# Twelve expert layers after attention on one NeuronCore: the first projection as seven block products in place of eight, tokens in two groups of 768

## The reference

```python
def _moe_ref(x, domain_probs, w1, w2) -> np.ndarray:
    ...
    p = domain_probs / (domain_probs.sum(-1, keepdims=True) + 1e-09)
    for e in range(E):
        h = np.maximum(x @ w1[e], 0.0)
        out += p[:, e:e + 1] * (h @ w2[e])

def _moe2_ref(x, w_gate, w1, w2) -> np.ndarray:
    ...
    logits = x @ w_gate
    logits = logits - logits.max()
    P = np.exp(logits)
    for _ in range(8):
        P /= P.sum(1, keepdims=True) + 1e-09
        P /= P.sum(0, keepdims=True) + 1e-09
        P *= N / E
    for e in range(E):
        h = np.maximum(x @ w1[e], 0.0)
        ye = h @ w2[e]
        out += P[:, e:e + 1] * ye
```

## Time and profile before

| | us |
|---|---|
| median of 3 runs | 1688.06 (1685.53 to 1688.75) |
| span of the profiled execution | 1684.4 |
| PE busy in it | 1651.6 |
| DVE busy | 489.4 |
| ACT busy | 322.8 |
| POOL busy | 35.3 |

### The profile page before, as it was taken

The page is one execution under the profiler, slowest core; times in us unless marked ns, Lnnn a source line. Parts: engine busy times, 40 slices in busy tenths (PEclk is TensorE's granted clock), DMA queues, the critical chain, the costliest instruction groups (busy, mean ns, idle before and its releaser), DMA issues.

```text
span 1684.4 us, 19145 instructions
## 1 busy us (share of the span) xinstructions
PE 1651.6 (98%) x8037; PEld 1363.8 (81%) x8037; DVE 489.4 (29%) x811; ACT 322.8 (19%) x551; POOL 35.3 (2%) x39
## 2 busy tenths in 40 slices
PE   6799999999999999999999999999999999999999
PEld 5778888888888887888888888888888888888887
DVE  5541321231231242272132132123123123123212
ACT  4631221121121131121121121112112112112110
POOL 2310000000000000000000000000000000000000
PEclk9799999999999999999999999999999999999999
DMA  8950020020020011002002002002002001100001
GB/s 188 147 167 1 0 100 1 1 100 0 0 99 0 0 50 51 1 3 98 1 0 100 0 0 100 0 0 100 0 0 99 0 0 59 40 0 0 8 17 50
DMA packets 50964, 66.56 MB, mean 40 GB/s; under 512 B 27880, under 2 KB 27880, under 8 KB 50928
## 3 DMA queue, kind: packets, MB, share of 16 engines
q1 hardware_dynamic: 50928, 66.04, 13.5%
HBM read 62.89 MB, written 3.15 MB: 39 GB/s over the span
## 4 chain that ended last, share of the span: by engine, by line
PE 94%; SPq 3%; issue 1%; DVE 1%; ACT 0%; DMA 0%; POOL 0%; POOLq 0%
PE banks L356 31%; PE banks L355 31%; PE banks L357 31%; SPq L187 1%; SPq L186 1%; PE banks L435 0%; DMA v_bd<-in_mem_v 0%; SPq L193 0%; SPq L189 0%; PE banks L316 0%; DVE acc L755 0%; PE banks L406 0%; PE banks L408 0%; PE banks L395 0%; SPq L169 0%
## 5 line engine op out<-in xcount | busy, mean ns | idle before, releaser
L706 DVE SCALAR_TENSOR_TENSOR h_lo<-banks,h_hi 128x512 fp32r<-128x512 f32 x288 | 199.0, 691 | 1130.0 <-ACT h_hi L571 1130.0
L356 PE MATMUL banks<-w_hi,h_hi 128*128 128x512 f32 x1152 | 453.8, 394 | 0.0
L355 PE MATMUL banks<-w_lo,h_hi 128*128 128x512 f32 x1152 | 451.9, 392 | 1.4 <-DVE x_lo L714 1.4
L355 PE MATMUL banks<-x_lo,w_hi 128*128 128x512 f32 x1152 | 448.8, 390 | 0.2
L356 PE MATMUL banks<-x_hi,w_hi 128*128 128x512 f32 x1152 | 448.2, 389 | 0.0
L357 PE MATMUL banks<-x_hi,w_lo 128*128 128x512 f32 x1152 | 447.9, 389 | 0.0
L357 PE MATMUL banks<-w_hi,h_lo 128*128 128x512 f32 x1152 | 447.4, 388 | 0.0
L571 ACT ACTIVATE h_hi<-banks 128x512 fp32r<-128x512 f32 x288 | 171.9, 597 | 1300.7 <-PE banks L357 1300.7
L355 PEld LDWEIGHTS banks<-w_lo,h_hi 128*128 128x128 f32 x1152 | 216.3, 188 | 50.9 <-DVE x_lo L714 1.8
L357 PEld LDWEIGHTS banks<-w_hi,h_lo 128*128 128x128 f32 x1152 | 216.2, 188 | 48.3
L355 PEld LDWEIGHTS banks<-x_lo,w_hi 128*128 128x128 f32 x1152 | 216.2, 188 | 47.3 <-DVE x_lo L744 0.7
(11 more groups left out here) (82 smaller groups left out, 297.4 us busy)
## 6 DMA issues: line engine op xcount, KB each, us to landing
w_raw<-in_moe_w SPq DMA_DIRECT2D x24, 2048.0 KB, 8.1
v_bd<-in_v SPq DMA_DIRECT2D x16, 308.0 KB
w_raw<-in_q SPq DMA_DIRECT2D x8, 384.0 KB, 5.0
w_raw<-in_k SPq DMA_DIRECT2D x8, 384.0 KB
out_x<-acc SPq DMA_DIRECT2D x12, 256.0 KB, 2.1
v_bd<-in_mem_v SPq DMA_DIRECT2D x16, 48.0 KB
v_bd<-in_v SPq DMA_DIRECT2D x16, 10.0 KB
v_bd<-in_v SPq DMA_DIRECT2D x16, 12.0 KB
```

The costliest lines, as they stand in the source:

```text
L355: pe.matmul(out_, lhs_hi, rhs_lo, start=start, stop=False)
L356: pe.matmul(out_, lhs_hi, rhs_hi, start=False, stop=False)
L706: dve.scalar_tensor_tensor(out=h_lo[:, f % 4, :], in0=h_ps[f % 4], scalar=0.0, in1=h_hi[:, f % 4, :].bitcast(F32), op0=ALU.max, op1=ALU.su ...
```

## The change

The first projection is done in blocks of 2 by 2: halves of the contraction (256 each), two chunks of hidden columns (128 each), halves of a batch (384 tokens each). With Strassen's scheme (Winograd's variant of it) seven block products give what eight would give; each product takes a sum or difference of weight blocks (`s`) as the stationary operand and one of token blocks (`t`) as the moving one. A quad is such a pair of hidden chunks for one batch: 42 matmuls with a moving operand of 384 columns, where the old order takes 48 for the same work with 384 each, or 36 with 512. 96 quads make up the program: batch 0 through the first mixture (quads 0 to 15), batch 1 (16 to 31), batch 0 through the second (32 to 63), batch 1 (64 to 95). All of it is written out, without loops.

- The seven products of a quad go to four banks of PSUM (`CHAIN`, `OPENS`): some are added by TensorE in the bank itself, and four partial sums are copied out by ScalarE (`keep_part`) and added back in PSUM by VectorE (`add`, 128x384) before the ReLU.
- GpSimd makes the sums of the weight blocks (`sum_s`, four operations of 256 columns a quad) and those of the tokens (`sum_t`, `sum_t4`, four of 768 columns a pass). ScalarE and VectorE split all seven weight blocks of a quad at once (1792 columns).
- `w1_raw` now holds one quad: the next quad's blocks are loaded with two transfers of 256 KB in rows of 512 bytes, when VectorE has split the last.
- The second projection is done by halves of an expert (4 chunks), in 24 pieces (tile, chunk) that are put between the products of the next two quads (`PIECES`). The output is accumulated twice an expert, in place of once.
- The chunks of expert 0 no longer stand in the attention. The logits are taken with the transposed rows as the stationary operand and 8 moving columns, 48 full-precision products in all.
- The eight rounds of the gates stand three to a quad, in quads 35 to 37.

```diff
+STATIONARY = (1, 2, 4, 3, 5, 0, 6)
+PRODUCTS = 7
+CHAIN = (0, 1, 0, 3, 0, 2, 3)
+OPENS = (True, True, False, True, False, True, False)
+PIECES = (2, 2, 1, 2, 2, 2, 1)
...
+    PASSES = 2 * B
+    FIRST = [0, EA, 2 * EA, 2 * EA + EB, 2 * EA + 2 * EB]
+    JOBS = FIRST[PASSES]
...
+        LAST_A = [4 * FIRST[b + 1] for b in range(B)]
+        TURNS = {}
+        for t in range(ST):
+            TURNS[LAST_A[0] + 2, t] = ("turn", 0, t)
+        TURNS[LAST_A[0] + 2, 6] = ("logits", 0, 0)
+        for t, (dq, i) in enumerate(((1, 0), (1, 1), (1, 2), (1, 4), (2, 0), (2, 1))):
+            TURNS[LAST_A[1] + dq, i] = ("turn", 1, t)
+        TURNS[LAST_A[1] + 2, 3] = ("logits", 1, 0)
+        SINK0 = LAST_A[1] + 3
...
+            def load_w1(quad):
+                n, j = quad // QUADS, quad % QUADS
+                src = weights(n)[0].rearrange("(c p) f -> p c f", p=P)
+                if quad:
+                    sp.wait_ge(s_lo_ready, quad)
+                for odd in (1, 0):
+                    f = 2 * j + odd
+                    at = 0 if odd else 2
+                    sp.dma_start(w1_raw[:, at:at + 2, :, :].rearrange("p a c f -> p (a c) f"),
+                                 src[:, :, f * P:(f + 1) * P]).then_inc(w1_loaded, 16)
+            def load_w2(m):
+                n, hf = m // HALVES, m % HALVES
+                src = weights(n)[1].rearrange("(c p) d -> p c d", p=P)
+                if m:
+                    sp.wait_ge(w2_lo_ready, 2 * m)
...
-                if u == 1:
-                    load_w1(0, a_w1[0], True)
-                if u == UNITS - 2:
-                    sp.wait_ge(q_ordered, UNITS)
-                    sp.wait_ge(k_ordered, UNITS)
-                    load_w2(0, a_w2[0], True)
+                if u == 2:
+                    load_w1(0)
...
+                if u == UNITS - 2:
+                    load_w1(1)
+            sp.wait_ge(q_ordered, UNITS)
+            load_w2(0)
+            for quad in range(ALLQ):
+                if quad + 2 < ALLQ:
+                    load_w1(quad + 2)
+                if quad % 2 == 1 and quad + 1 < ALLQ:
+                    load_w2((quad + 1) // 2)
+                if quad == QUADS * FIRST[3] + 2:
+                    for t in range(ST):
+                        store(0, HALVES * FIRST[3] - 1, t)
+            for t in range(ST):
+                store(1, ALLM - 1, t)
             sp.wait_ge(stored, 16 * TILES)
...
+            def sum_s(quad):
+                a21, a22, a11, a12, s1, s2, s3, s4 = [w1_raw[:, i, :, :] for i in range(8)]
+                pool.wait_ge(w1_loaded, 32 * (quad + 1))
+                pool.tensor_tensor(out=s1, in0=a21, in1=a22, op=ALU.add).then_inc(s_step, 1)
+                pool.tensor_tensor(out=s3, in0=a11, in1=a21, op=ALU.subtract)
+                pool.wait_ge(s_step, 2 * quad + 1)
+                pool.tensor_tensor(out=s2, in0=s1, in1=a11, op=ALU.subtract).then_inc(s_step, 1)
+                pool.wait_ge(s_step, 2 * quad + 2)
+                pool.tensor_tensor(out=s4, in0=a12, in1=s2, op=ALU.subtract).then_inc(s_summed, 1)
+            def sum_t(p):
+                b = p % B
+                if p == 0:
+                    pool.wait_ge(x_taken, PAIRS)
+                else:
...
+                one, two = as_block(t_one[:]), as_block(t_two[:])
+                pool.tensor_tensor(out=one, in0=block_of(b, 0, 1), in1=block_of(b, 0, 0),
+                                   op=ALU.subtract).then_inc(t_summed, 1)
+                pool.wait_ge(t_summed, 4 * p + 1)
...
+                if u == 5:
+                    sum_s(0)
+                if u == 6:
+                    sum_t(0)
+                if u == 7:
+                    sum_t4(0)
+            sum_s(1)
+            for quad in range(ALLQ):
+                for p in range(1, PASSES):
+                    if quad == QUADS * (FIRST[p] - 1):
+                        sum_t(p)
+                    if quad == QUADS * FIRST[p] - 1:
+                        sum_t4(p)
+                if quad + 2 < ALLQ:
+                    sum_s(quad + 2)
+                if quad == SINK0 - 1:
+                    pool.wait_ge(lmax_ready, 1)
+                    pool.partition_all_reduce(gmax, lmax, P, RED.max).then_inc(gmax_ready, 1)
+                if SINK0 <= quad < SINK0 + 3:
+                    for it in range(3 * (quad - SINK0), min(3 * (quad - SINK0) + 3, SINKHORN)):
+                        pool.wait_ge(csum_ready, it + 1)
+                        pool.partition_all_reduce(ctotal, csum, P, RED.add).then_inc(ctotal_ready, 1)
...
+            def product(quad, i):
+                p = pass_of(quad // QUADS)
+                if i == 0:
+                    pe.wait_ge(s_lo_ready, quad + 1)
+                    if quad:
+                        pe.wait_ge(h_lo_ready, 4 * (quad - 1) + 2)
+                    else:
+                        pe.wait_ge(x_taken, UNITS)
+                if quad == QUADS * FIRST[p]:
+                    pe.wait_ge(t_lo_ready, PRODUCTS * p + t_place(p, i) + 1)
+                if i == 2:
+                    pe.wait_ge(part_copied, 4 * quad + 1)
+                if i == 3 and quad:
+                    pe.wait_ge(h_lo_ready, 4 * (quad - 1) + 4)
+                if i == 4:
+                    pe.wait_ge(part_copied, 4 * quad + 2)
+                if i == 6:
+                    pe.wait_ge(part_copied, 4 * quad + 3)
+                s, par = STATIONARY[i], quad % 2
+                for c in range(2):
+                    mm = in_three(c_ps[CHAIN[i]], s_hi[par][:, s, c, :], s_lo[par][:, s, c, :], t_hi[:, i, c, :],
+                                  t_lo[:, i, c, :], OPENS[i] and c == 0, c == 1, chained=not OPENS[i])
+                mm.then_inc(prod_done, 1)
+            def down(m, t, f):
+                y, par = m * ST + t, m % 2
+                if t == 0 and f == 0:
+                    pe.wait_ge(h_lo_ready, 8 * (m + 1))
+                    pe.wait_ge(w2_lo_ready, 2 * (m + 1))
+                if f == 0 and y >= 3:
+                    pe.wait_ge(y_taken, y - 2)
+                ts = slice(t * P, (t + 1) * P)
+                mm = in_three(y_ps[y % 3], h_hi[par][:, f, ts], h_lo[par][:, f, ts], w2_hi[par][:, f, :],
+                              w2_lo[par][:, f, :], f == 0, f == 3)
+                if f == 3:
+                    mm.then_inc(y_summed, 1)
...
+            for quad in range(ALLQ):
+                m = quad // 2 - 1
+                piece = 12 * (quad % 2)
+                for i in range(PRODUCTS):
+                    if (quad, i) in TURNS:
+                        what, b, t = TURNS[quad, i]
+                        if what == "turn":
+                            turn_rows(b, t)
+                        else:
+                            logits(b)
+                    product(quad, i)
+                    for _ in range(PIECES[i]):
+                        if m >= 0:
+                            down(m, piece // 4, piece % 4)
+                        piece += 1
+            for t in range(ST):
+                for f in range(4):
+                    down(ALLM - 1, t, f)
...
+            def split_s(quad):
+                act.wait_ge(s_summed, quad + 1)
+                if quad >= 2:
+                    act.wait_ge(prod_done, PRODUCTS * (quad - 1))
+                act.activation(s_hi[quad % 2][:], w1_raw[:, 1:PRODUCTS + 1, :, :], ACT.Copy).then_inc(s_hi_ready, 1)
...
+            def keep_part(quad, j):
+                act.wait_ge(prod_done, PRODUCTS * quad + (1, 3, 4, 5)[j])
+                act.activation(part[:, j, :], c_ps[(0, 0, 3, 0)[j]], ACT.Copy).then_inc(part_copied, 1)
+            def hidden(quad, k):
+                act.wait_ge(c_added, 4 * quad + k + 1)
+                act.activation(hidden_at(h_hi, quad, k), c_ps[BLOCKS[k][0]], ACT.Relu).then_inc(h_hi_ready, 1)
...
+                keep_part(quad, 0)
+                next_tokens(quad, 0)
+                if quad + 1 < ALLQ:
+                    split_s(quad + 1)
...
+                hidden(quad, 0)
+                take_turned(quad, 2)
+                keep_part(quad, 1)
+                next_tokens(quad, 2)
+                take_turned(quad, 3)
+                split_w2(quad // 2, quad % 2)
+                keep_part(quad, 2)
+                next_tokens(quad, 3)
...
+                keep_part(quad, 3)
+                next_tokens(quad, 4)
+                hidden(quad, 1)
+                take_turned(quad, 5)
+                hidden(quad, 2)
+                next_tokens(quad, 5)
+                hidden(quad, 3)
...
+            def split_s(quad):
+                dve.wait_ge(s_hi_ready, quad + 1)
+                dve.tensor_tensor(out=s_lo[quad % 2][:], in0=w1_raw[:, 1:PRODUCTS + 1, :, :],
+                                  in1=s_hi[quad % 2][:].bitcast(F32), op=ALU.subtract).then_inc(s_lo_ready, 1)
...
+            def add(quad, k):
+                dve.wait_ge(prod_done, PRODUCTS * quad + (2, 5, 6, 7)[k])
+                dve.wait_ge(part_copied, 4 * quad + (1, 4, 4, 4)[k])
```

(39 more changed lines are left out.)

641 lines of the change are left out of this document (245 added, 396 removed).

## The result

The changed kernel takes 1726.8 us (median of 4 runs, 1724.46 to 1730.89), the kernel before in the same comparison 1688.4 (1685.53 to 1689.24): a ratio of 1.0233, with an interval of 1.022 to 1.0247. It is 2.3% slower, where 1683 and a small gain were forecast, and it lies outside the range of 1660 to 1708. The profiled execution has a span of 1729.1 us.

What follows compares the result with a forecast made beforehand. PE was taken to bound the kernel. Start 151, 93 quads 1444, half waits 12, gates 31, passes with transposes and logits 19, last pieces 16.5 plus wait 1.3, end 3.7: 1679 us span, 1683 median against 1688; range 1660 to 1708.

Steps and rivals of the forecast that it cites:

- The pitch: Start-to-start time of first-projection matmuls with 384 columns on PE: 173.4 ns, so 699 us for 4032.
- the steady wait: PE waits for the last hidden block of a half: 0.27 us on every second quad, 12 us in all.
- the start: Attention and first quads: last `attend` at 103 us, first product at 109, quad 3 at 151.
- the ring of the gates: Quads 35 to 37: splits, transfer, GpSimd sums, reductions and rounds wait in a circle, 26.4 us a quad, 31 us lost.
- one of the prediction's own signs of being wrong: The prediction is wrong if PE's clock falls outside the start and the gates; no size given.
- Rivals 1: First-projection products: a matmul's excess grows with its columns, pitch 170.0 ns, 14 us less, 1669 us; chance 0.22.
- 4 (188): First-projection products: stationary loads bound the pitch at 188 ns, 59 us more, 1742 us; chance 0.08.
- The steady quad: Each ordinary quad on PE: 42 x 0.1734 + 36 x 0.2291 = 15.53 us.
- The passes: Last quad of three passes: seven more splits give VectorE 16.5 us of work in 15.5, 8 us lost in all.
- rival 3: VectorE's chain at each second quad is longer than it looks, waits of 0.5 to 0.8 us, 1707 us; chance 0.18.
- The logits: 96 logit passes on PE at 0.06 to 0.11 us each: 6 to 10 us, taken as 6.
- From span to median: Median run time taken as 3.7 us over the profiled span, as before, so 1679 of span gives 1683.

Runs made afterwards that it cites:

- b4_vfirst: Changed kernel with quad 1's weights loaded behind the last unit's v, not ahead of it; first product starts at 93.6 us, against 110.3 in the changed kernel.
- b2_logits: Changed kernel with logits spread out, one tile at a time in quad 19, two in quad 34; those quads and quad 18 take 6.3 us less, 4.8 in all.

## Why the prediction was wrong, step by step

The pitch, the steady wait and the start held. What failed is the price of the rare places, above all the ring of the gates, and two costs that the sum had at nothing: the change of GpSimd's code and the lower clock behind waits and in the logits. The last is one of the prediction's own signs of being wrong, a clock that falls outside the start and the gates (quads 16, 18, 32, 34 and 64).

- **The pitch of the product: right.** The timeline of PE in quad 48 has 174 ns from start to start, and of the matmuls in quads 44 to 61 most start 173 or 174 ns after the one before. Rivals 1 (170.0) and 4 (188) fall by the same rows.

```profile
942.18 0.33 PE L439 MATMUL banks<-t_lo,s_hi 128*128 128x384 f32 x1
942.35 0.33 PE L440 MATMUL banks<-t_hi,s_hi 128*128 128x384 f32 x1
942.53 0.34 PE L441 MATMUL banks<-t_hi,s_lo 128*128 128x384 f32 x1
942.88 0.50 PE L439 MATMUL banks<-w_lo,h_hi 128*128 128x512 f32 x1
```

- **The steady quad: 15.67, not 15.53.** The step "a quad is 42 x 0.1734 + 36 x 0.2291" priced each matmul among its own kind. Where the length changes, some 20 ns more go for each change and return, seven times a quad. 0.14 x 93 is 13 us.
- **The wait at every second half: right.** 0.27 us were forecast, 15.94 less 15.67 measured, and the last two rows above show it (0.35 from product to piece in place of 0.17).
- **The start: right in size.** `attend` at 103.3 for 103, the first product at 110.3 for 109, quad 3 at 152.8 for 151. The first product of the same attention lies anywhere from 104.3 to 110.3, so a hit within 2 us is in part luck. `b4_vfirst` shows the cause as told: a wait ahead of the v transfers.
- **The gates: 41.6 us, not 31.** The step that failed is the ring's list, which gave 26.4 us a turn (its terms add up to 26.6). Quads 36 and 37 take 30.1 and 29.6. The list had 5.2 us from the split to the landing and a reduction of 1.0. From the split's end to the first sum it is 3.8 (702.8 to 706.6; a transfer lands in 3.2, the median on the page after), and from the last sum's end to the reduction's 6.4 (709.5 to 715.9), three times: the change of GpSimd's code, which the list did not have. In the kernel before, this change lay in 44 us of idle time ahead of its only series of reductions (MODIFY_POOL_CONFIG at 642.9, the first reduction at 686.9), so no row of waiting showed it. By the Trainium skill (GPSIMD Engine Reference, section "2.1 Instruction dispatch") the first call of a newly loaded GpSimd routine pays about 6 us; the traces agree with 5.5 to 6.0. They have 6.7 to 7.1 for the way back. The piece of POOL's order shown ahead of the prediction held the hint: a row "L372 ISA" with no operands ahead of each three reductions, and "L307 ISA" behind.
- **The passes: 21.6 us, not 8.** I summed VectorE's load (16.5 against 15.5) where the order decided. In each of the three quads, 2.5 of the 4.7 us of waiting went with three splits out of the way and all but 0.5 with five. The lock with GpSimd, which the prediction named and left to rival 3, holds VectorE up by 1.7 us in the same chain; what it alone is worth was not tried. And each wait was followed by 1.9 to 2.6 us lost to the half clock, which no term had.
- **The logits: 16.3 us, not 6.** Two batches of 48 passes at 0.111 us are 10.6. I had taken the lower end of 6 to 10, without a reason. The other 5.7 are the clock, about what `b2_logits` gives back.
- **Transposes: right**, 5.3 for 5.
- **From span to median: wrong by 6.** The profiled execution was 3.7 us under the median before and is 2.3 above it now. The runs settle half of it. Every execution for which both numbers are known takes 1.8 to 2.1 us more than its own span. So of the 3.7, some 1.8 were this, and some 1.9 that the profiled execution was a quick one; the changed kernel's was the longest of its four (1730.9 against a median of 1726.8). The step that failed is carrying the luck of one execution over to another kernel. Starts that vary by 6 us are the likely reason for the spread; that was not tried.

The terms missed are 13 + 10.6 + 13.6 + 10.3 and 2 for the start, 49.5 of the 50.1 us between 1679 and 1729.1. **Rival 3**, the one on the slow side, gave 1707 and named the wrong place: its chain of seven steps was as long as forecast. The slow side came about by 13 us in the steady quads (the changes of length) and by 35 at places that happen two or three times each. The range had no room for those, since the rare places were priced by sums of work.

What stays open: why a change of length costs some 20 ns, and whether the clock's cost behind a wait can be had for less than a filler. Neither was tried further.

## What to carry to other kernels

Where a change brings waits back to an engine that had none, price each wait twice, for itself and for the clock behind it, and do so for the rare stretches too: here 93 steady quads were off by 1%, and some ten others by 35 us. Count an engine's changes from one kind of code to another as operations of their own, above all where a change puts two kinds in turns that were apart before. And when a restructured kernel comes out slower, look at the rare quads before giving it up: four repairs of a few lines each, plus another grouping of the pieces, turned 2.3% slower into 3.3% faster.
